# V's block sums beside the first keys, first weights rounded on GpSimd and split during the attention, fill products right behind the lists

## What is computed

```python
# attention: 2 batches x 8 heads x 768 tokens x 64
k_sum = k.reshape(B, H, nb, block, D).max(axis=3)      # 24 blocks of 32 keys: maxima
v_sum = v.reshape(B, H, nb, block, D).mean(axis=3)     # and means of V ("V's sums")
scores = [window of +-15 keys | q @ k_sum + log(32)]
x = softmax(scores) @ [v | v_sum]                      # 1536 tokens x 512
# mixture 1: top 2 of 8 experts by noisy logits (x@w_gate + log1p(exp(x@w_noise))*noise)
#   out += gate * (relu(x @ w1[e]) @ w2[e])            # 512 -> 1024 -> 512
# mixture 2: tokens with x @ w_skip > 0 go to their best expert, x + gate * y; the others keep x
```

## Time and profile before

| | |
|---|---|
| median of 3 runs | 670.94 us (670.56 to 673.47) |
| the profiled execution: its own time | 678.62 us |
| its span, first to last instruction | 676.1 us |
| its mean granted TensorE clock | 0.957 |
| PE busy | 625.1 us, 92% of the span |
| DVE, ACT, POOL busy | 364.5, 297.0, 234.5 us |
| chain that ended last, by engine | PE 82%, DVE 6%, DMA 5%, issue 3% |

### The profile page before, as it was taken

One profiled execution on the slowest core, in us unless ns is written; L12 is line 12 of the kernel. 1 busy time (PEld: TensorE's weight loads), 2 busy tenths in 40 slices (PEclk: granted clock), 3 DMA queues, 4 the chain that ended last, 5 costly groups with the idle time before them and its releaser, 6 DMA issues.

```text
span 676.1 us, 13586 instructions
## 1 busy us (share of the span) xinstructions
PE 625.1 (92%) x4071; PEld 557.6 (82%) x4071; DVE 364.5 (54%) x712; ACT 297.0 (44%) x538; POOL 234.5 (35%) x221
## 2 busy tenths in 40 slices
PE   6798863999999999999999999999699999999994
PEld 5577761799999999999999999996478888788883
DVE  4667739354644536454463545431675577556641
ACT  1667824143433434343343444324264576545531
POOL 2557102300725528072462706406023123231130
PEclk9999955899999999999999999999699999999998
DMA  9999931551572927448292654887196759567321
GB/s 318 342 282 265 306 144 52 177 188 63 141 207 54 273 61 187 124 120 231 53 255 74 174 147 89 223 297 165 20 328 221 231 191 343 162 201 249 63 47 16
DMA packets 57634, 119.81 MB, mean 177 GB/s; under 512 B 13588, under 2 KB 13972, under 8 KB 57568
## 3 DMA queue, kind: packets, MB, share of 16 engines
q1 hardware_dynamic: 39424, 94.59, 42.7%
q0 software_dynamic: 14304, 23.93, 16.9%
q10 hardware_dynamic: 3840, 0.49, 0.4%
HBM read 103.51 MB, written 23.50 MB: 188 GB/s over the span
## 4 chain that ended last, share of the span: by engine, by line
PE 82%; DVE 6%; DMA 5%; issue 3%; ACT 1%; POOLq 0%; POOL 0%; DVEq 0%; SPq 0%; ACTq 0%
PE bank L843 22%; PE bank L837 21%; PE bank L951 19%; PE bank L826 2%; DMA xg<-x_moe,ix_take 2%; PE bank L806 2%; PE bank L733 2%; PE bank L745 2%; PE bank L685 2%; PE bank L705 2%; PE bank L716 2%; PE bank L967 1%; DMA out<-y_sb,ix_put 1%; PE bank L755 1%; PE bank L667 1%
## 5 line engine op out<-in xcount | busy, mean ns | idle before, releaser
L1580 DVE TENSOR_TENSOR w_lo<-stage,w_hi x120 | 141.6, 1222 | 22.8 <-ACT w_hi L1076 18.7
L1076 ACT CAST w_hi<-stage x120 | 119.7, 1050 | 9.0 <-PE bank L951 8.9
L843 PE MATMUL bank<-unit_hi,w_hi 128*128 128x416 f32 x256 | 92.6, 362 | 0.0
L837 PE MATMUL bank<-tok_hi,w_hi 128*128 128x416 f32 x256 | 90.5, 354 | 0.6 <-DVE tok_lo L1790 0.6
L1185 ACT ACTIVATE unit_hi<-bank 128x416 fp32r<-128x416 f32 x64 | 33.2, 519 | 129.8 <-PE bank L837 117.2
L843 PE MATMUL bank<-unit_lo,w_hi 128*128 128x416 f32 x256 | 90.1, 352 | 0.0
L1838 DVE SCALAR_TENSOR_TENSOR unit_lo<-bank,unit_hi 128x416 fp32r<-128x416 f32 x64 | 37.9, 592 | 96.7 <-ACT unit_hi L1185 71.8
L837 PE MATMUL bank<-tok_hi,w_lo 128*128 128x416 f32 x256 | 89.7, 351 | 0.0
L843 PE MATMUL bank<-unit_hi,w_lo 128*128 128x416 f32 x256 | 89.7, 350 | 0.0
L1394 POOL DMA_INDIRECT x_more<-more_out,ix_put x32 | 52.1, 1627 | 42.1 <-DVE more_out L1809 26.3
L1406 POOL DMA_INDIRECT x_moe<-rows_out,ix_put x32 | 55.3, 1727 | 9.8 <-issue 9.8
(11 more groups left out here) (163 smaller groups left out, 1080.7 us busy)
## 6 DMA issues: line engine op xcount, KB each, us to landing
stage<-in_moe_w SPq DMA_DIRECT2D x128, 512.0 KB, 5.4
v_win<-in_v SPq DMA_DIRECT2D x24, 198.0 KB, 9.1
v_raw<-in_v SPq DMA_DIRECT2D x6, 528.0 KB, 13.4
x_moe<-rows_out SPq DMA_DIRECT2D x12, 260.0 KB, 4.0
kt<-in_k SPq DMA_DIRECT2D x8, 384.0 KB, 9.8
q_ring<-in_q SPq DMA_DIRECT2D x6, 512.0 KB, 10.2
x_att<-x_sb POOLq DMA_DIRECT2D x12, 256.0 KB, 5.5
x_part<-x_moe SPq DMA_DIRECT2D x4, 768.0 KB, 8.1
```

The lines of the kernel that those rows point to most:

```text
L837: last = eng.matmul(ps_unit[f % 2][:, 0:W], w, x, start=(i == 0), stop=(i == len(mine) - 1))
L843: last = eng.matmul(ps_out[chunk][:, 0:W], w[:, WC // 2 + f, chunk * P:(chunk + 1) * P], h[:, f % UNITS, :], start=(f == 0 and i == 0), st ...
L1076: eng.copy(piece(w_hi[n % SETS], j), stage[:, j, :]).then_inc(s_hi, 1)
L1580: eng.tensor_tensor(piece(w_lo[n % SETS], j), stage[:, j, :], piece(w_hi[n % SETS], j).bitcast(F32), ALU.subtract)\
```

## The change

- `vsum` is no buffer of its own: ACT writes V's sums straight into the first window of the batch in `v_win` (with a wait on `s_pv` for batch 1); POOL copies them from there to the other seven windows.
- The "v" jobs stand ahead of `turn_p` on PE and of `empty_pt` on ACT. The 8 fill transposes of step 2 are gone.
- POOL copies the keys of both windows of a tile before it copies their maxima.
- DVE makes batch 1's maxima at steps 3 (two), 4 and 5 rather than 4 to 7; its four casts of constants move from step 2 to step 9.
- SP loads the second piece of queries and batch 1's keys two windows earlier, and the constants of those casts behind them rather than ahead of all windows. ACT issues its last four DMAs only when batch 0's keys have landed.
- POOL rounds all eight first pieces, at tiles 6 to 11; ACT rounds none. DVE splits five pieces at steps 15, 17, 19, 21, 23 and three behind its last tile, ahead of the routing; none behind the lists.
- PE makes 11 fill products in place of 12, and waits for `s_last_gates` behind the transposes of the gathered rows, not ahead of the fill.

```diff
--- before.py
+++ after.py
@@ -252,7 +252,8 @@
         v_win = sb_in(att, "v_win", [KEYS, WR, VROW])
-        vsum = [sb_in(att, f"vsum{b}", [NSUM, VROW]) for b in range(BATCH)]
+        vsum = [v_win[0:NSUM, b * NWIN % WR] for b in range(BATCH)]
         s_sb = sb_in(att, "s_sb", [P, 2, GH, KEYS])
@@ -376,7 +377,6 @@
         s_first = sem("s_first")
-        s_fhi_down = sem("s_fhi_down")
         s_fhi = sem("s_fhi")
@@ -458,11 +458,13 @@
         DVE_BLOCKS = 2
-        KEY_MAXIMA = {4: (0,), 5: (1,), 6: (2,), 7: (3,)}
+        KEY_MAXIMA = {3: (0, 1), 4: (2,), 5: (3,)}
...
                 at_step.setdefault(s, []).append(("x", t))
+        for s in at_step:
+            at_step[s].sort(key=lambda job: job[0])
         jobs = [j for s in range(-1, LAST + 1) for j in at_step.get(s, [])]
@@ -480,6 +482,8 @@
             elif job[0] == "v":
+                if job[1]:
+                    eng.wait_ge(s_pv, NG * ((job[1] * NWIN - WR) // 2 + 1))
                 dst, src = vsum[job[1]][:, job[2] * VC:(job[2] + 1) * VC], ps[0:NSUM, 0:VC]
@@ -568,13 +572,14 @@
             load_values(0)
-            eng.dma_start(c_early[:, casts - early:], const[:, casts:]).then_inc(s_casts, 16)
             for t in range(NT):
...
                     load_window(w)
-                if t == 1:
+                if t == 0:
                     load_queries(1)
                     load_keys(1)
+                elif t == 1:
+                    eng.dma_start(c_early[:, casts - early:], const[:, casts:]).then_inc(s_casts, 16)
                 elif t == 3:
@@ -685,7 +690,7 @@
-            IDLE = {0: 16, 1: 8, 2: 8, STEPS + 3: 8}
+            IDLE = {0: 16, 1: 8, STEPS + 3: 8}
@@ -725,7 +730,11 @@
                         eng.wait_ge(s_win[w % WR], 16 * (w // WR + 1))
-                        eng.wait_ge(s_vw, w // NWIN * WR + min(w % NWIN + 1, WR))
+                        if w % NWIN == 0:
+                            for hh in range(2):
+                                wait_job(eng, ("v", w // NWIN, hh))
+                        else:
+                            eng.wait_ge(s_vw, w // NWIN * (WR - 1) + min(w % NWIN, WR - 1))
                 for i in range(GH):
@@ -888,12 +897,12 @@
                 eng.wait_ge(s_first, PIECES // 2)
-                eng.wait_ge(s_last_gates, 2)
-                keep_warm(12, ps_turn)
+                keep_warm(11, ps_turn)
                 for t in range(PARTS):
...
                     keep_warm(0 if t == PARTS - 2 else 3, ps_turn)
+                eng.wait_ge(s_last_gates, 2)
                 for e in range(E):
@@ -1001,6 +1010,9 @@
                     scores(s // NG)
+                for job in at_step.get(s, []):
+                    if job[0] == "v":
+                        do_job(job)
                 if 0 <= s - TURN_LAG < STEPS:
@@ -1014,7 +1026,8 @@
                 for job in at_step.get(s, []):
-                    do_job(job)
+                    if job[0] == "x":
+                        do_job(job)
             for t in (NT - 2, NT - 1):
@@ -1076,27 +1089,24 @@
             eng.dma_start(c_early[:, 0:casts - early], const[:, early:casts]).then_inc(s_const, 16)
+            eng.preload_act_table_set("natural_log_exp_and_others")
+            eng.wait_ge(s_k[0, PAIRS - 1], 16)
             eng.dma_start(c_late[:, P:early], const[:, P:early]).then_inc(s_late, 16)
...
-            def round_first(j):
-                eng.wait_ge(s_loaded, j + 1)
-                eng.copy(piece(w_hi[0], j), stage[:, j, :]).then_inc(s_fhi_down, 1)
-            ROUND_AT = (20, 22, 24, 26)
-            eng.preload_act_table_set("natural_log_exp_and_others")
             for s in range(LAST + 1):
...
                     exponentials(s - 1)
+                for job in at_step.get(s, []):
+                    if job[0] == "v":
+                        empty_job(eng, job)
                 if 0 <= s - TURN_LAG < STEPS:
...
                 for job in at_step.get(s, []):
-                    empty_job(eng, job)
-                if s in ROUND_AT:
-                    round_first(PIECES // 2 + ROUND_AT.index(s))
+                    if job[0] == "x":
+                        empty_job(eng, job)
             eng.wait_ge(s_gt[0], NT)
@@ -1298,12 +1308,22 @@
                     eng.wait_ge(s_score, NG * ((w - WKR) // 2 + 1))
-                place = k_win[:, w % WKR]
-                copied = eng.tensor_copy(place[:, :, NSUM:KEYS], kt[b][:, :, start:start + WK])
-                if w % NWIN < WKR:
-                    eng.wait_ge(s_ksum, PAIRS * (b + 1))
-                    copied = eng.tensor_copy(place[:, :, 0:NSUM], ksum[b][:])
-                copied.then_inc(s_kw, 1)
+                copied = eng.tensor_copy(k_win[:, w % WKR, :, NSUM:KEYS], kt[b][:, :, start:start + WK])
+                if w % NWIN >= WKR:
+                    copied.then_inc(s_kw, 1)
+            def maxima_beside(w):
+                b = w // NWIN
+                eng.wait_ge(s_ksum, PAIRS * (b + 1))
+                eng.tensor_copy(k_win[:, w % WKR, :, 0:NSUM], ksum[b][:]).then_inc(s_kw, 1)
+            def keys_of_tile(t):
+                for w in (2 * t, 2 * t + 1):
+                    window_of_keys(w)
+                for w in (2 * t, 2 * t + 1):
+                    if w % NWIN < WKR:
+                        maxima_beside(w)
@@ -1323,7 +1343,7 @@
                     eng.wait_ge(s_pv, NG * ((w - WR) // 2 + 1))
-                eng.tensor_copy(v_win[0:NSUM, w % WR], vsum[b][:]).then_inc(s_vw, 1)
+                eng.tensor_copy(v_win[0:NSUM, w % WR], vsum[b]).then_inc(s_vw, 1)
@@ -1335,22 +1355,21 @@
-            ROUND = 6
-            for w in range(WKR):
-                window_of_keys(w)
+            ROUND = {6: (0,), 7: (1,), 8: (2,), 9: (3, 4), 10: (5, 6), 11: (7,)}
+            for t in range(WKR // 2):
+                keys_of_tile(t)
             for t in range(NT):
...
                 for w in (2 * t, 2 * t + 1):
-                    if w % NWIN < WR:
+                    if 0 < w % NWIN < WR:
                         sums_beside(w)
-                for w in (2 * t + WKR, 2 * t + WKR + 1):
-                    if w < BATCH * NWIN:
-                        window_of_keys(w)
+                if t + WKR // 2 < NT:
+                    keys_of_tile(t + WKR // 2)
                 if t >= 2:
                     store_x(t - 2)
-                if ROUND <= t < ROUND + PIECES // 2:
-                    round_first(t - ROUND)
+                for j in ROUND.get(t, ()):
+                    round_first(j)
             for t in (NT - 2, NT - 1):
@@ -1583,16 +1602,13 @@
-                if j < PIECES // 2:
-                    eng.wait_ge(s_fhi, j + 1)
-                else:
-                    eng.wait_ge(s_fhi_down, j - PIECES // 2 + 1)
+                eng.wait_ge(s_fhi, j + 1)
                 eng.wait_ge(s_vp_pool, BATCH)
...
-            SPLIT_AT = (17, 19, 21, 23)
+            SPLIT_AT = (15, 17, 19, 21, 23)
             steps = [0]
@@ -1960,7 +1976,7 @@
                     block_maxima(1, i)
-                if s == 2:
+                if s == 9:
                     eng.wait_ge(s_casts, 16)
@@ -1970,13 +1986,13 @@
                     split_first(SPLIT_AT.index(s))
+            for j in range(len(SPLIT_AT), PIECES):
+                split_first(j)
             eng.wait_ge(s_router, 16 * 3)
...
             index_lists(0)
-            for j in range(PIECES // 2, PIECES):
-                split_first(j)
             first_mixture()
```

## The result

The changed kernel takes **666.89 us** (median of 4 runs, 666.22 to 667.79) where the kernel before, with one more run beside it, takes 670.99 (4 runs, 670.56 to 673.47). The ratio on record is 0.9895, with a 95% interval of 0.9849 to 0.9941: faster by about 1%. The quotient of these two medians alone is 0.9939, at the upper edge of the interval. The forecast was 661.8 us, so 5.1 us too low; 666.89 lies outside the range of 656 to 666.5 by 0.4 us.

The account below looks back on a forecast made before the run. PE bounds the kernel and is full from about 130 us; time can be won before the first expert's product. Terms -1.9 - 0.2 - 0.5 + 0.1 + 0.4 - 0.9 - 6.1 = -9.1 from 670.94 give 661.8 us, range 656 to 666.5.

Parts of the forecast that it names:

- The start, -1.9 and -0.2: First tiles: earlier V sums bring the third tile's scores forward 1.9 us; earlier key copies and queries bring first scores 0.2.
- Batch 1's maxima, -0.5: Attention's middle: moving two of DVE's four maxima to step 3 shortens tiles of 5.26 us towards 4.95, saving 0.5 us.
- casts at step 9, +0.1: Attention's middle: DVE's casts of constants, moved to step 9, cost 0.1 us there; their old place was covered.
- One more tile with a split, +0.4: Attention, step 15: one more tile carries a DVE split, 5.38 us instead of 4.95; ends 0 and +1.6.
- the tile of 5.38 already has a long split: Attention's splits: reason given against adding 1.2 us for two more splits at 1.81 us beside POOL's rounding.
- The tail, -0.9: Attention's tail: without ACT's rounding of 1.05 us, PE's gap of 1.39 us shrinks to some 0.5; saves 0.9 us.
- no idle of over 0.6 us near 79: Attention's tail: a sign that would show the forecast right, PE idling at most 0.6 us near 79 us.
- The three splits behind the last tile: End of attention: three splits, 3.66 us on DVE, are covered by the last logits, transposes and noise scale.
- Behind the lists, -6.1: Lists to first expert's product: earlier fill and gathers bring that product to 122.5 us, saving 6.1; ends -4.0 and -7.4.
- Behind the first product, 0: From about 130 us on: PE is full, so an earlier start moves everything earlier; no term was given.
- The clock holds in the tail: Rival, attention's tail: with the gap cut, PE may stay at 2.4 GHz until the last logits, giving 656.8 us; chance 0.24.
- The clock falls early: Rival, first tiles: a pause brings 1.2 GHz, which would not come back; up to 698 us; chance 0.04.

Follow-up runs that it names:

- base_again: The kernel before, unchanged, in a second profiled execution; that execution took 672.67 us.
- weights_alone: The kernel before with only the change's weights part (POOL rounds all eight pieces, splits ahead of the routing, early fill), start as before; ratio 0.9912 to before.
- round_ahead: The changed kernel with POOL's rounding of the first weights ahead of its store of x instead of behind it; 664.05 us, ratio 0.9873 to before.
- after_again: The changed kernel, unchanged, in a second profiled execution; median 666.03 us, ratio 0.9884 to before.
- after: The changed kernel itself, in its first measurement and profile; 666.89 us, ratio 0.9895 to before.

## Why the forecast was off

**What it was set against.** The sum was applied to the median of three runs, 670.94. Four later sets of runs of the same kernel have medians of 673.39 to 674.06. Against those, the ratios of 0.9884 and 0.9895 are gains of 7.1 to 7.8 us, where the sum said 9.1; against the three runs the gain reads 4.1. So of the 5.1 us, 2.5 to 3.1 come from a base of three runs that lay low, and 2.0 to 2.6 from the terms (1.1 to 1.8 by the repeat's median of 666.03). Whether the three lay low by chance or by their chip no run shows. The profile used for the terms erred the other way: 7.7 above that median. Its span is 6.0 us longer than base_again's, and 3.9 of these lie between tile 11 and the lists, where its clock was at half for longer.

**The start, -1.9 and -0.2: right, the second too small.** Tile 0 to 2 fell by 1.74 to 1.78 us, tile 0 itself by 0.65 to 1.6, though two kernels with the same start had it at 10.97 and 11.08. DVE waited 0.16 and 0.26 us for the keys at step 3, not 1.

**Batch 1's maxima, -0.5:** -0.4 in one trace, 0 in the other. What the tiles gained they gave back to waits for v_win and q_ring.

**Batch 1's V sums: a missing term.** The forecast had "casts at step 9, +0.1" for tiles 5 to 6. It became +1.7 to +2.2: 0.54 to 0.67 of it is PE's wait for POOL's sum, whose bytes do not come earlier, and 0.97 to 1.63 the pause. The cast was wrongly priced from its old place beside nothing (3.6 us in place of 0.22), and by luck that cost PE nothing.

**"One more tile with a split, +0.4", ends 0 and +1.6: the step that failed most.** In weights_alone, which has no pause, the splits cost 1.5 us between tiles 6 and 11 (26.87 against 25.36). The failed reasoning was "the tile of 5.38 already has a long split": a split beside one rounding is held 0.6 us and nearly fits, a split beside two is held 1.55 and makes a tile of 6.23. round_ahead, which takes most of the meeting away, needs 25.44 us for the same tiles, with a pause of 0.49 us among them. The page that was cited (The Trainium skill, "GPSIMD Engine Reference", Key points) pointed to the upper end, and the upper end is what was measured. The stretch lost more than that, 2.3 us in after_again and 4.8 in after: the rest is the pause, 0.77 and 2.41 us, with half a clock behind it in after. For that the sum had no term.

**The tail, -0.9:** -1.45, and not for the reason given. PE's idle time of 1.39 us did not shrink to 0.5. It is 1.54 us, in after before 81.07 and in after_again before 79.36, behind the split that the second pair of roundings holds; "no idle of over 0.6 us near 79" failed. What the tail gained is the clock: base_again ran at 0.55 and 0.60 from 80 to 84 us, and after and after_again at 1.00 from 80 to 90. That the number came close is luck. Why the clock held over a gap of 1.54 us, when it fell behind one of 1.39, stays open. In round_ahead the gap is 0.58 us, and the tail takes 12.84 us in place of 13.66. **The three splits behind the last tile:** hidden, as said; last logits to lists is 12.56 and 12.57 us, where base_again has 12.58.

**Behind the lists, -6.1: right.** -5.7 and -5.6. The clock rose where it was said to, and PE waits for the gathers' landings by under 0.5 us each.

**Behind the first product, 0:** -1.2 to -1.4, not looked for.

**Rivals.** "The clock holds in the tail" came true (1.00 over 80 to 90 us in both traces of after), but most of it lay in the base already: before's tail takes 17.65 us, base_again's 15.11, after's 13.66. "The clock falls early" asked for a clock that would not come back with this work; it fell at 55 us in the profiled run of after, behind the pause of 2.41 us, and was back at 1.00 by 60. That claim was wrong, and so was the price hung on it.

## What to carry to other kernels

Before an instruction is moved to GpSimd, or a cast on VectorE to another step, look for what the other engine does at that very moment: here two operations released by the same event met in every tile, and the order on one queue (the rounding ahead of the store) took most of the meetings apart. When a start is brought forward, check the DMA share of the stretch that follows: here, at 1.0, the bytes did not come earlier, and the wait turned up at the next tile that needed them. A term that comes out near its number may still have another cause, so look at the wait that it was to remove. And take the base from more than three runs when the gain sought is 1%.

## What was not expected of the hardware

- A 128x128 cast on DVE takes 0.22 us alone and took 3.58 beside a 3.62 us sum on POOL; a split of two SBUF inputs ends 1.07 to 1.09 us behind the rounding that it meets. Before, the two meetings that the profile had (1.81 us) showed only its mild form.
- The hold works both ways: two roundings that take 2.03 us took 2.96 behind a split that had begun.
- PE pauses 0.2 to 2.4 us at fixed places of its instruction stream, 122 matmuls apart, while transfers keep the DMA engines busy; eight matmuls more ahead moved one pause by eight. Not every place shows one, nor every execution.
- After the half clock of 55 to 58 us, a stretch of the same small products had 2.4 GHz again by 60 us.
